# A delta-rule recurrence before two gated layers: the state is grown and then multiplied by a decay mask, the lead-in is written out by hand, and its first triangular solve runs on VectorE

## The reference

```
y[t]    = r[t] @ state
Sa      = state @ a[t]
state   = state * w[t] (per column) - outer(Sa, b[t]) + outer(v[t], k[t])
```

## Time and profile before

| | |
|---|---|
| median of 3 runs | 1127.23 us (1122.25 to 1128.94) |
| profiled execution | 1123.35 us, span 1121.6 us |
| busy in the span | PE 93%, PE weight load 77%, DVE 46%, ACT 31%, POOL 26% |
| recurrence | from 0 to about 444 us |
| the two layers | from about 446 us to the end |

### The profile page before, as it was taken

How to read it: one execution, slowest core, us unless ns; L and a number is a source line. 1 busy time by engine, 2 the same in 40 slices (tenths; PEclk the granted TensorE clock), 3 DMA queues, 4 the chain that set the end, 5 groups by cost and what they waited for, 6 DMA issues and landing times. The chain is left out here.

```text
span 1121.6 us, 21667 instructions
## 1 busy us (share of the span) xinstructions
PE 1039.6 (93%) x8872; PEld 867.0 (77%) x8872; DVE 514.6 (46%) x875; ACT 352.0 (31%) x732; POOL 291.3 (26%) x527
## 2 busy tenths in 40 slices
PE   6577999899989996999999999999997999999998
PEld 3445778787778885788888888888885888888886
DVE  6726776567774443553323223332225543342432
ACT  3213544444444442432222222222223211111111
POOL 4788869588785500000000000000000000000000
PEclk7766999899999998899999999999998999999999
DMA  7632345455522225630000200000002100000000
GB/s 173 157 78 68 94 112 136 95 135 131 125 71 71 72 65 136 177 97 0 29 1 23 60 1 1 1 0 0 0 0 64 45 24 23 1 24 8 16 23 23
DMA packets 53247, 66.23 MB, mean 59 GB/s; under 512 B 19944, under 2 KB 40680, under 8 KB 53160
## 3 DMA queue, kind: packets, MB, share of 16 engines
q1 hardware_dynamic: 53160, 65.00, 22.7%
HBM read 57.12 MB, written 7.86 MB: 58 GB/s over the span
## 5 line engine op out<-in xcount | busy, mean ns | idle before, releaser
L1144 DVE TENSOR_TENSOR hid<-gate,gbank 128x512 f32<-128x512 f32 x72 | 49.5, 688 | 204.1 <-ACT gate L1090 204.1
L875 PE MATMUL mbank<-x_hi,w_hi 128*128 128x512 f32 x324 | 127.7, 394 | 6.7 <-DVE w_lo L1329 6.7
L392 POOL TENSOR_TENSOR inv_step<-lab 128x30 f32<-128x30 f32 (+9 forms) x180 | 120.0, 667 | 35.9 <-DVE lab L682 22.2
L875 PE MATMUL mbank<-x_hi,w_lo 128*128 128x512 f32 x324 | 127.0, 392 | 0.0
L1090 ACT ACTIVATE gate<-gbank 128x512 f32<-128x512 f32 x72 | 43.1, 598 | 226.4 <-PE gbank L875 226.4
L400 POOL TENSOR_TENSOR lab<-lab,inv_step 128x30 f32<-128x30 f32 (+9 forms) x180 | 110.4, 613 | 14.1
L1346 DVE TENSOR_TENSOR hid<-hid,mbank 128x512 f32<-128x512 f32 x72 | 49.5, 687 | 97.3 <-PE mbank L875 94.2
L875 PE MATMUL gbank<-x_hi,g_hi 128*128 128x512 f32 x216 | 84.9, 393 | 8.0 <-DVE v_lo L1124 8.0
L875 PE MATMUL mbank<-x_lo,w_hi 128*128 128x512 f32 x216 | 85.3, 395 | 0.0
L1045 PE MATMUL gbank<-h_hi,o_hi 128*128 128x512 f32 x216 | 84.1, 390 | 1.0 <-DVE h_lo L1150 1.0
L875 PE MATMUL gbank<-x_hi,g_lo 128*128 128x512 f32 x216 | 84.8, 392 | 0.0
(11 more groups left out here) (130 smaller groups left out, 2015.0 us busy)
## 6 DMA issues: line engine op xcount, KB each, us to landing
lent_w<-kb_in SPq DMA_DIRECT2D x12, 720.0 KB, 6.7
r_m<-rm_in SPq DMA_DIRECT2D x24, 360.0 KB, 3.7
lent_x<-w_in SPq DMA_DIRECT2D x10, 742.5 KB, 6.1
a_t<-a_in SPq DMA_DIRECT2D x12, 360.0 KB, 4.7
r_t<-r_in SPq DMA_DIRECT2D x11, 360.0 KB, 6.6
vu_rows<-v_in SPq DMA_DIRECT2D x24, 160.0 KB, 6.1
out<-o_sb SPq DMA_DIRECT2D x6, 640.0 KB, 3.2
x<-y_t SPq DMA_DIRECT2D x48, 60.0 KB, 3.2
```

The lines of the kernel that those rows point to most:

```text
L392: product = nc.gpsimd.tensor_tensor(part, column, row, op=ALU.mult)
L875: last = mm(out, w, x, start=n == 0, stop=n == len(seq) - 1)
L1144: nc.vector.tensor_tensor(hid[:, m % 2, :], gate[:, m % 2, :], p_val[m % 2][:, :], op=ALU.mult).then_inc(hid_done, 1)
```

## The change

1. `inc`: the product with the identity is gone. The increments alone are summed in PSUM; DVE adds the old state (into `s_new`), waits for its own result, and multiplies it by `decay_mask`. This mask (decay times block mask, two buffers) is written by ACT in a new step `dm`, four operations for each group. `s_t` is cleared by POOL at the start. PE's wait ahead of the increments is for the addition (`grown`).
2. `LEAD_IN` and turn 0 are replaced by one list `LEAD`. Its first solve runs on DVE, at once after the first transposition, followed by the transposition back. The scans of pairs 2 to 4 stand behind it. For pairs 2, 3 and 4 (`BY_POOL`) the scaling of a, k and b is done by POOL, in its place in the list. The second solve (step `lab` of pair 2) remains on POOL.
3. `TURN`: the second `kb` step stands ahead of `gr` 5 and of the `am` steps; the second `am` step stands behind the third `kb` step; `gr` 4 stands ahead of the second `inc`.
4. SP: v of pairs 0 and 1 is loaded before w, a, kb of pair 2; a of pairs 3 and 4 is loaded earlier.

```diff
-    ("t2", 2), ("kb", 0), ("inc", 1), ("gr", 4), ("scale_a", 0), ("ts", 2), ("ty", 1), ("gr", 5), ("am", 0), ("am", 1),
-    ("scale_kb", 0), ("kb", 1),
-    ("inc", 2), ("y", 2), ("kb", 2), ("scale_kb", 1), ("inv", 0),
+    ("t2", 2), ("kb", 0), ("gr", 4), ("inc", 1), ("scale_a", 0), ("ts", 2), ("dm", 2), ("ty", 1), ("kb", 1), ("gr", 5),
+    ("am", 0), ("scale_kb", 0),
+    ("inc", 2), ("y", 2), ("kb", 2), ("am", 1), ("scale_kb", 1), ("inv", 0),
...
+LEAD = (
+    ("scan", 0, 0), ("scan", 0, 1), ("decay", 0, 0), ("scale_a", 0, 0), ("am", 0, 0), ("scale_kb", 0, 0),
+    ("scale_kb", 0, 1), ("am", 0, 1),
+    ("ga", 0, 0), ("ga", 0, 1), ("am", 0, 2), ("scan", 1, 0), ("ga", 0, 2), ("ga", 0, 3), ("scan", 1, 1),
+    ("decay", 1, 0), ("ga", 0, 4), ("ga", 0, 5), ("scale_a", 1, 0), ("am", 1, 0), ("scale_kb", 1, 0),
+    ("scale_kb", 1, 1), ("am", 1, 1), ("kb", 0, 0),
+    ("ga", 1, 0), ("ga", 1, 1), ("am", 1, 2), ("ga", 1, 2), ("ga", 1, 3), ("kb", 0, 1), ("ga", 1, 4), ("ga", 1, 5),
+    ("vx", 0, 0), ("vx", 0, 1), ("vx", 0, 2), ("kb", 0, 2), ("lab", 0, 0), ("dm", 0, 0), ("kb", 1, 0), ("dm", 0, 1),
+    ("kb", 1, 1), ("kb", 1, 2),
+    ("scan", 2, 0), ("t1", 0, 0), ("scan", 2, 1), ("t1", 0, 1), ("low", 0, 0), ("decay", 2, 0), ("scale_a", 2, 0),
+    ("scale_kb", 2, 0), ("scale_kb", 2, 1), ("t1", 0, 2), ("low", 0, 1), ("t2", 0, 0), ("am", 2, 0), ("low", 0, 2),
+    ("t2", 0, 1), ("inc", 0, 0), ("t2", 0, 2), ("am", 2, 1), ("scan", 3, 0), ("inc", 0, 1), ("dm", 0, 2),
+    ("scan", 3, 1), ("ga", 2, 0), ("ga", 2, 1), ("inc", 0, 2), ("am", 2, 2), ("decay", 3, 0), ("ga", 2, 2),
+    ("ga", 2, 3), ("scale_a", 3, 0), ("scale_kb", 3, 0), ("scale_kb", 3, 1), ("ga", 2, 4), ("ga", 2, 5), ("am", 3, 0),
+    ("kb", 2, 0), ("am", 3, 1), ("kb", 2, 1), ("scan", 4, 0), ("ga", 3, 0), ("ga", 3, 1), ("kb", 2, 2), ("am", 3, 2),
+    ("ga", 3, 2), ("ga", 3, 3), ("ga", 3, 4), ("ga", 3, 5), ("lab", 2, 0), ("scan", 4, 1), ("decay", 4, 0),
+    ("scale_a", 4, 0), ("am", 4, 0), ("am", 4, 1), ("kb", 3, 0), ("scale_kb", 4, 0), ("kb", 3, 1),
+    ("scale_kb", 4, 1), ("kb", 3, 2),
+)
+
+BY_POOL = (2, 3, 4)
...
@@ gpsimd
-                    elif name == "lab":
-                        solve_block(k // 2)
+                    elif name == "lab" and k > 0:
+                        pool.wait_ge(labt_done, k // 2 + 1)
+                        solve_block(pool, nc.gpsimd, k // 2 - 1, solve)
+                    elif name == "scale_a" and k in BY_POOL:
+                        pool.wait_ge(lab_kept, kept)
+                        scale_a(pool, nc.gpsimd, k)
+                        pool.wait_ge(at_done, k + 1)
...
@@ vector
             def next_state(k, g):
-                hd = HD[g]
-                dve.wait_ge(ds_done, 3 * k + g + 1)
-                for at in range(4):
-                    s = 4 * g + at
-                    last = nc.vector.scalar_tensor_tensor(
-                        s_t[0:hd, s, 0:hd], p_ds[0:hd, at * hd:at * hd + hd], decay[0:hd, k % 4, s:s + 1],
-                        diag_mask[0:hd, :, :].rearrange("e i d -> e (i d)")[:, 0:hd], op0=ALU.mult, op1=ALU.mult)
-                last.then_inc(s_done, 1)
+                n, hd = 3 * k + g, HD[g]
+                state = s_t[0:hd, 4 * g:4 * g + 4, 0:hd]
+                new = s_new[0:hd, 0:4 * hd].rearrange("e (s f) -> e s f", s=4)
+                if n == 0:
+                    dve.wait_ge(s_zero, 1)
+                dve.wait_ge(ds_done, n + 1)
+                dve.wait_ge(s_done, n)
+                nc.vector.tensor_tensor(new, p_ds[0:hd, 0:4 * hd].rearrange("e (s f) -> e s f", s=4), state,
+                                        op=ALU.add).then_inc(grown, 1)
+                dve.wait_ge(grown, n + 1)
+                dve.wait_ge(dm_done, n + 1)
+                nc.vector.tensor_tensor(state, new, decay_mask[0:hd, n % 2, :, 0:hd], op=ALU.mult).then_inc(s_done, 1)
...
                     elif name == "lab":
                         turn_lab(k // 2)
+                        if k == 0:
+                            dve.wait_ge(labt_done, 1)
+                            solve_block(dve, nc.vector, 0, solve_0)
+                            turn_inv(0)
...
@@ scalar
+            def mask_decay(k, g):
+                n, hd = 3 * k + g, HD[g]
+                if n >= 2:
+                    act.wait_ge(s_done, n - 1)
+                mask = diag_mask[0:hd, :, :].rearrange("e i d -> e (i d)")[:, 0:hd]
+                if k == 0:
+                    act.wait_ge(scale_done, 4)
+                for at in range(4):
+                    s = 4 * g + at
+                    last = copy(decay_mask[0:hd, n % 2, at, 0:hd], mask, decay[0:hd, k % 4, s:s + 1])
+                last.then_inc(dm_done, 1)
```

More of the change, by code:

```diff
@@ L94, in steps @@
             continue
-        if name == "ts" and k == 0 or name == "inc" and k == PAIRS - 1:
+        if name in ("inc", "dm") and k == PAIRS - 1:
             continue
         yield name, k, x
-TURNS = range(FIRST, PAIRS + 2)
+TURNS = range(PAIRS + 2)
 TR_USE = {}
@@ L309, in _ @@
             load_kb(1)
+            for k in range(2):
+                load_v(k)
             load_w(2)
@@ L335, in _, with solve_block, step, scale_a @@
             sp.wait_ge(st_y[1], 16 * 5 * (PAIRS // 2))
+        def solve_block(eng, ops, n, done):
+            at = [n * N_SOLVE]
+            def step(ins):
+                at[0] += 1
+                ins.then_inc(done, 1)
+                eng.wait_ge(done, at[0])
+            for s in range(1, C - 1):
+                rows, cols = C - 1 - s, s
+                part = inv_step[:, 0:rows * cols].rearrange("p (t j) -> p t j", t=rows)
+                column = lab[:, s + 1:C, s:s + 1].broadcast_to([128, rows, cols])
+                row = lab[:, s:s + 1, 0:cols].broadcast_to([128, rows, cols])
+                product = ops.tensor_tensor(part, column, row, op=ALU.mult)
+                if s == 1:
+                    at[0] += 1
+                    product.then_inc(done, 1)
+                    step(ops.memset(lab[:, :, :].rearrange("p t s -> p (t s)")[:, ::C + 1], -1.0))
+                else:
+                    step(product)
+                rest = lab[:, s + 1:C, 0:cols]
+                step(ops.tensor_tensor(rest, rest, part, op=ALU.subtract))
+            assert at[0] == (n + 1) * N_SOLVE
+        def scale_a(eng, ops, k):
+            eng.wait_ge(ld_a[k % 5], 16 * (k // 5) + 16)
+            eng.wait_ge(scale_done, 2 * k + 2)
+            eng.wait_ge(at_done, k)
+            ops.tensor_tensor(a_t[:, k % 5], a_t[:, k % 5], scale_t[:, k % 6], op=ALU.mult).then_inc(at_done, 1)
+        def scale_kb(eng, ops, k, half):
+            kb = kb_t[:, k % 2].rearrange("e s (j h t) -> e s j h t", j=2, h=2)[:, :, :, half, :]
+            eng.wait_ge(kbt_done, 2 * k + half)
+            if half == 0:
+                eng.wait_ge(ld_kb[k % 2], 16 * (k // 2) + 16)
+                eng.wait_ge(prod_done, 2 * k + 2)
+                by = products(1)[:, :, 0, C - 1::-1]
+            else:
+                eng.wait_ge(tail_done, k + 1)
+                by = tail_inv[:, :, :]
+            ops.tensor_tensor(kb, kb, bc(by, 2, 2), op=ALU.mult).then_inc(kbt_done, 1)
         @block.gpsimd
@@ L743, in _ @@
                         decay_factors(k)
-                    elif name == "scale_a":
-                        scale_a(k)
-                    elif name == "scale_kb":
-                        scale_kb(k, x)
+                    elif name == "scale_a" and k not in BY_POOL:
+                        scale_a(dve, nc.vector, k)
+                    elif name == "scale_kb" and k not in BY_POOL:
+                        scale_kb(dve, nc.vector, k, x)
         @block.scalar
```

91 lines of the change are left out of this document (30 added, 61 removed), and 7 rows, old and new, of tables (LEAD_IN, TURN).

## The result

The changed kernel takes 1165.77 us (1165.65 to 1166.88) against 1124.74 us (1120.83 to 1128.94) in the same comparison: ratio 1.0347, 95% interval 1.031 to 1.0384. The profiled execution has a span of 1165.2 us, 43.6 us more than the one of before.

A forecast was written before the change was run, and what follows sets the result against it. The prediction took POOL's solve as the bound; 28 us late after the lead-in, +9 for the mask product and -2 for turn 10 made +35 on 1123.35 us, 1158.4, stated as 1160 us, range 1145 to 1176.

The forecast's parts named there:

- What bounds the kernel: Steady turns: POOL's solve sets each 62.4 us cycle of two turns; the other engines have only 1.2 us to spare.
- The identity product is worth nothing in turns 2 to 9: Steady turns: 2.2 us of PE per turn for the product, 4.0 with two waits, hidden by POOL's solve.
- The mask product: State step in solves 3 to 6: two SBUF inputs clash with POOL, +2.3 us per solve, +9 us (0 to 14).
- The masks on ACT: Each turn: ACT's mask copies take 3.3 us, but cost the kernel zero.
- The lead-in up to the second transposition: Start: DVE's solve saves 25 us, spent on work behind it; second transposition at 92 to 93 us, give or take 5.
- The open solve: Second solve: pair 4's scaling queues behind it on POOL, other engines stop, `vx` of turn 1 at 139 us, +32.4 us.
- What comes back: After the second solve: turn 1 gains 2.5 us, turn 2 up to its transposition to the solve 2 us.
- The slow clock: Rival, later turns: PE waits longer for the solve, falls to 1.2 GHz, three more times 3.1 us, 1168 us; chance 0.15.
- pair 4 not held: Rival, second solve: pair 4's scaling isn't held by the solve, so turn 1 starts about 103 us, 1130 us; chance 0.04.
- faster: Rival, steady turns: PE sets them after all, eight turns give 4.0 us each, 1117 us or 1111 us; chance 0.03.

The follow-up runs named there:

- e7: The kernel before with 15 of the 30 steps of every solve left out and the old state step kept: 1101.02 us.
- e2: The kernel before with the new state step alone (no identity product, mask from ACT), its own lead-in and order: 1135.19 us, ratio 1.0077.
- e4: The kernel before with the moved steps of the turn alone: 1134.01 us, ratio 1.0058.
- e8: e7 with the new state step (no identity product), half of every solve's steps still left out: 1096.83 us.
- e6: The changed kernel with the state sum written back to PSUM and multiplied from there, PE waiting for the product: 1156.27 us.
- e1: The changed kernel with pair 4 scaled on DVE instead of POOL: 1142.12 us, ratio 1.0139.
- e9: The changed kernel with no scaling on POOL, DVE scaling every pair: 1143.42 us.
- e3: The changed kernel with the old state step (identity product, four DVE operations, no mask step): 1163.19 us.
- e5: e4 with PE kept busy by spare products while it waits for the end of POOL's solve and DVE's transposition: 1119.50 us, ratio 0.9937.
- e11: e5 with each solve split between POOL and DVE, plus the new state step with its sum in PSUM: 1120.68 us.
- e12: The changed kernel with pair 4 scaled on DVE, the state sum in PSUM and spare products in PE's waits: 1133.22 us, ratio 1.0051.

## Why the prediction was right

The forecast was 1160 us in 1145 to 1176; it is 1165.8. By its steps:

- **What bounds the kernel.** Right: half solves (e7) shorten a cycle by 0.6 to 2 us and no more, and with whole solves neither the removed product (e2) nor the moved steps (e4) gained anything.
- **The identity product is worth nothing in turns 2 to 9.** Right (e2), and even with half solves it is worth little there (e8). In turn 10 I had booked -2 us; the stretch behind the last solve changed by -0.3. There the granted clock is 0.85 over the stretch from 426.5 us to the layers, against 0.94 before.
- **The mask product.** Right in kind, and the size was off: I took 2.3 us for each of four solves; it is 1.1 to 1.3 for three and 2.0 for the last, 5.6 instead of 9 us. I had scaled from one row beside a longer operation (+0.65 us); beside the real one the row shows +0.28. One product in each later solve begins while POOL is in a step and waits itself (0.92 to 1.02 instead of 0.66 us), which costs DVE and not POOL.
- **The masks on ACT.** Zero was right for POOL's bound; ACT is busy 28.9 to 29.5 instead of 22.5 to 23.2 us in a solve stretch, and nothing is seen to wait for the masks; e6 has the same masks and solve stretches of 46.0 to 46.4 us.
- **The lead-in up to the second transposition.** Solve on DVE: 22.0 us measured from 36.3 to 58.4, 21.5 predicted. From there I had 34 us and it is 39: I had priced POOL's scaling at 1.5 us, it is 1.7 to 1.8 us alone, and it also blocks DVE, which I left out (1.71 instead of 0.66 us, and a wait of 2.65 us). The second transposition came 5 us after my 92 to 93 us, at the edge of the 5 us that I had allowed.
- **The open solve.** Right in every link. Solve 36.5 us (37 predicted), from its end to `vx` of turn 1 7.4 us (7 predicted), `vx` at 143.5 us (139, the 5 us from above). e1 took the cause away and the time with it.
- **What comes back.** Turn 1 takes 28.2 instead of 31.1 us, -2.9 (-2.5 predicted), turn 2 up to its transposition 17.0 instead of 18.4, -1.4 (-2).
- **The slow clock.** I had it as a rival at +9 us, with a chance of 0.15, and left it out of the sum. +5.0 us came in the free stretches of the profiled execution, 4.8 of them in one, and 1165.8 us lies nearer to this rival's 1168 than to my 1160. But its mechanism is not what happened. It has PE done earlier and waiting longer for the solve; in the changed kernel PE waits 0.4 to 1.6 us behind the transpositions back, no longer than before, and the clock fell 4 us ahead of the one at 367 us. e9 shows the same four times. The rival's mechanism is that of e3, e4 and e5, with waits of 3.6 us and more. Without the spare products a free stretch is anything from 15.6 to 20.6 us, and what makes the clock fall ahead of that wait stays open.

In the profiled executions the change costs 43.6 us where my sum had 35. The errors partly cancel: lead-in +4.5, clock +5, last turn +2, layers +0.8, mask product -3.4. By the medians it costs 41.0 us, and 1160 us meant 32.8. That the forecast itself is off by 6 us only is in part luck: the kernel before came out at 1124.7 us beside the changed one instead of 1127.2. The last two rivals, pair 4 not held and faster, are out by the rows of the gap.

## What to carry to other kernels

Before work is moved to an idle engine, look at what its queue will be doing at that place in the order: three operations of under 2 us cost 24 us here because they stood behind a long chain, and everyone waited for them. If an engine that is not the bound is let through faster, it arrives earlier at the same wait. In e4 PE then waited 3.7 to 6.4 us, came out at half its clock or fell to it at once, and the stretch behind the wait, which is PE's, got longer. Fill such a wait, as e5 does, but let the filling end before what PE waits for is there: in e11 and e12 it ran on and cost 6 to 7 us. A product with two SBUF inputs on VectorE is not free beside a busy GpSimd (1.5 to 2.1 us of the solve for six of them); with one input in PSUM the same products no longer lengthened it.

## What was not expected of the hardware

- Spare products in a wait of 4 to 6 us are worth 2.6 to 4.4 us each time: the free stretches of e4 and e5 differ by 3.5 us on average, with no other difference between the kernels.
- A long wait is not needed for the clock to fall: in the changed kernel and in e9 it fell in or behind a wait of 1.4 us in each of six turns, and in e9 the four falls ahead of a transposition back each left it at 1.2 GHz for 17 us.
- Less PE work can make PE's work slower: without the identity product the granted clock in the stretches of the third and fourth solve is 0.90 and 0.87 in the changed kernel and 0.93 and 0.91 in e2, against 1.00 and 0.96 before and 1.00 in e3. It need not: e12, with the same state step and spare products in the waits, has 1.00 in both. Where POOL's solve covers it, the lower clock costs nothing there (e6: 0.89 and 46.4 us). What decides it in the middle of a turn stays open; the wait of 1.4 us is the best candidate.
- The clash between DVE and POOL goes both ways and hits small steps hardest: DVE's 30-element step is 0.19 us alone and 0.37 us beside POOL's copies; DVE's 0.66 us product became 1.71 us beside a POOL scaling of 1.80 us.
